# Attention, routed experts and a gated MLP on one core: where a cast load and five gathers stand on GpSimd's queue, the order of row numbers and tables, and the first slot's rows by blocks of 128

## The chip, the cores and the metric

The kernel runs on one core of one Trainium2 chip. The metric is the device time of one execution in microseconds (us); less is better. Engines are called as in the profile: PE is TensorE (its weight loads are PEld), DVE is VectorE, ACT is ScalarE, POOL is GpSimd, SP is SyncE. A q behind a name (POOLq, SPq) is the queue in which that engine issues DMAs.

## The reference

Three layers, all in float32, with 4 batches of 576 tokens:

```python
# 1. attention with a threshold, 8 heads of 64
scores = scale * q @ k.T
scores = where(scores >= max(scores) - tau, scores, -1e9)
x = softmax(scores) @ v                       # reshaped to [2304, 512]
# 2. each token goes to one of 8 experts (512 -> 1024 -> 512)
logits = norm(x) @ norm(expert_emb).T / moe_tau
e = argmax(logits);  gate = softmax(logits)[e]
y = gate * (relu(x @ w1[e]) @ w2[e])
# 3. a dense layer with a mish gate (512 -> 2048 -> 512)
h = y @ w_in;  out = (h * tanh(softplus(h))) @ w_out
```

## The kernel before, in words

**Stages.** By the trace, attention runs to about 294 us, routing to about 323 us, the experts to about 660 us, and the dense layer to the end.

**Slots.** Routing sorts the 2304 tokens by expert into slots of 128 rows. There are SLOTS = 25 of them; with these inputs the experts 0 to 7 begin at slots 0, 2, 5, 7, 9, 12, 15 and 19. The number of each row is worked out on DVE and PE (`sel`, `tid`, a matmul over 18 tiles into the bank at INV0) and becomes `inv_i` (L1437 and L1438). POOL then fetches the rows of each slot from `x_tok` in DRAM by an indirect DMA, `gather(s)` (L629).

**One slot on PE** (`slot(i)`): `m1(i)`, 24 blocks of matmuls of 512 columns in all (2 halves, 4 blocks of k, 3 passes: high x high, high x low, low x high; L1111 to L1113), then `t_x(i + 1)`, four transposes of the next slot's rows (L1107), then `m2(i - 1)` (24 matmuls), then `t_h(i)` (8 transposes). The three passes are how float32 products are formed from float32r operands: each operand is a high part (a copy into float32r) and a low part (the difference). For the rows, ACT makes `xth` (`high_x`, L840) and DVE makes `xtl` (`low_x`, L1484).

**The weights.** Each expert's weights have 16 chunks of 128x512 in 4 quarters; quarters 0 and 1 are w1, 2 and 3 are w2. The high part comes by a casting DMA of 1 MB, `load_quarter(e, par, i)` (L603), issued by POOL. The low part needs the raw chunk too: SP loads it into one of 4 `stage` buffers (L475), each once POOL has used that buffer's chunk before (`w_split`), and POOL subtracts (`low_quarter`, `low_parts`, L592). There are two sets of buffers for the high parts, so expert e's quarters 0 and 1 may load once all m1 of expert e - 2 are done, and its quarters 2 and 3 once all m2 of it are.

**The order on POOL** behind attention is written out by hand: the cast loads of expert 1's quarters 1 to 3, low parts of its quarters 1 and 2, the 15 gathers of slots 0 to 14 (they wait for `placed`), 3 gathers that wait for `gates_kept` (the slots' gates, written by DVE at L1477 when PE has done the matmuls of `gsel`, L1163), and then for each expert e from 2 on `next_expert(e)`:

```python
wait m1_done (all slots before expert e - 1)
load_quarter(e, 0);  load_quarter(e, 1)
if e == 2: gather(18), gather(19)
low_quarter(e - 1, 3);  low_quarter(e, 0)
wait m2_done (all slots before expert e - 1)
load_quarter(e, 2);  load_quarter(e, 3)
low_quarter(e, 1);  low_quarter(e, 2)
```

Between `next_expert(2)` and `next_expert(3)` stand the 5 gathers of slots 20 to 24. PE's `m1` of an expert's slots waits for `w_split` of its first 8 chunks, the last of which is the end of `low_quarter(e, 1)`.

**ps** is PSUM: 8 banks of 512 columns. The transposed rows of a slot go to columns 0 to 511, `m1` writes 512 to 1535, `t_h` 1536 to 2559, `m2` 2560 to 3071.

Of the kernel before, what the change touches and what calls it, by code (L numbers as in the profile page):

```python
# [16 lines left out]
ALU = mybir.AluOpType  # L17
ACT = mybir.ActivationFunctionType
# [57 lines left out]
HEAD = 4  # L76
YW = D + 1
# [5 lines left out]
def build(nc, qT, kT, v, tau, embT, moe_tau, w1, w2, w_in, w_out, out):  # L83
# [335 lines left out]

    LG0 = 2048  # L420
# [107 lines left out]
    def _(g):  # L528
# [93 lines left out]
        for i in range(1, QUARTERS):  # L622
            load_quarter(1, 1, i)
        for i in range(1, 3):
            low_quarter(1, 1, 1, i)

# [15 lines left out]
        def next_expert(e, par, n):  # L642

            first = g.value_load(start_i[0:1, bass.ds(e - 1, 1)], min_val=1, max_val=SLOTS)
            g.wait_ge(m1_done, g.snap(first * 2))
            g.sem_inc(pool_passed, 1)
            load_quarter(e, par, 0)
            load_quarter(e, par, 1)
            if isinstance(e, int) and e == 2:
                for s in range(FAR, AHEAD):  # L650
                    gather(s)
            low_quarter(e - 1, 1 - par, n - 1 + par, 3)
            low_quarter(e, par, n, 0)
            g.wait_ge(m2_done, first)
            g.sem_inc(pool_passed, 1)
            load_quarter(e, par, 2)
            load_quarter(e, par, 3)
            low_quarter(e, par, n, 1)
            low_quarter(e, par, n, 2)

        next_expert(2, 0, 2)
        for s in range(AHEAD, SLOTS):
            gather(s)
# [90 lines left out]
    def _(act):  # L754
# [82 lines left out]
        def high_x(i):  # L837
            act.wait_ge(tx_done, i + 1)
# [33 lines left out]
        high_x(0)  # L872
# [58 lines left out]
    def _(pe):  # L931
# [160 lines left out]
        def t_x(i):  # L1092
# [11 lines left out]
            wait(pe, xth_ready, i)  # L1104
            wait(pe, xtl_ready, i)
# [12 lines left out]
        def m1(i, e):  # L1118
            pe.wait_ge(w_split, e * CH_E + CH_E // 2)
            pe.wait_ge(xtl_ready, i + 1)  # L1120
            par = pe.snap(e % 2)
            for h in range(2):
                wait(pe, relu_done, 2 * i - 1 + h)
                for k in range(KD):
                    o = k * F + h * 512
# [133 lines left out]
    def _(dve):  # L1259
# [169 lines left out]
        for t in range(NT):  # L1429
            dve.tensor_scalar(sel[:, t, :], lane_b[:, :], prow[:, t:t + 1], None, ALU.is_equal).then_inc(sel_ready, 1)  # L1430
        dve.tensor_copy(start_i[:, :], start[:, :])
# [4 lines left out]
        dve.wait_ge(inv_mm, 1)  # L1436
        link(dve.tensor_copy(idp[:, :], ps[:, INV0:INV0 + SLOTS]))  # L1437
        dve.scalar_tensor_tensor(inv_i[:, :], ps[:, INV0 + SLOTS:INV0 + 2 * SLOTS], float(P), idp[:, :], ALU.mult,  # L1438
                                 ALU.add).then_inc(placed, 1)
# [41 lines left out]
        def low_x(i):  # L1481

            dve.wait_ge(xth_ready, i + 1)
# [26 lines left out]
        low_x(0)  # L1510
# [110 lines left out]
```

## Time and profile before

| | |
|---|---|
| time of 3 runs | 1074.81, 1074.88, 1077.37 us; median 1074.88 us |
| profiled execution | 1076.51 us, of which the span of instructions is 1074.9 us |
| PE busy | 1026.1 us, 95% of the span |
| DVE, ACT, POOL busy | 627.3, 505.8, 587.3 us |
| mean granted PE clock | 0.982 of 2.4 GHz |

The time of the profiled execution is 1.6 us longer than its span, and 1.6 us longer than the median of the three runs. Busy shares say where an engine works, not where it holds up the end; a row that ends in [t <-X] says that the engine sat idle for t before it and that X ended this.

### The profile page before, as it was taken

To read this page: it belongs to the slowest core of one execution; us is meant where nothing else is said; L and a number is where in the kernel's file an instruction comes from. 1 tells how busy PE (TensorE), PEld (TensorE's weight loads), DVE (VectorE), ACT (ScalarE), POOL (GpSimd) and SP (SyncE) were. 2 spreads that over 40 slices of the span, in tenths; PEclk is the share of its full clock that TensorE was granted. 3 is DMA by queue.
4 is the path that set the end of the run, shared out by engine and by line. 5 is a ranking of instruction groups with operands and counts; after the bars stand their busy time and mean duration, and the time that the engine had idled before them with its cause. 6 is when DMAs were issued, how large, how long until landed. Compare 5 with 4: busy or idle time off the path is not lost.

```text
span 1074.9 us, 20987 instructions
## 1 busy us (share of the span) xinstructions
PE 1026.1 (95%) x6712; PEld 852.0 (79%) x6712; DVE 627.3 (58%) x1484; ACT 505.8 (47%) x1020; POOL 587.3 (55%) x672
## 2 busy tenths in 40 slices
PE   7999999999956999899999998999999999999996
PEld 5777777777735888688888887999999999999995
DVE  6998989888763222122222226766676676666663
ACT  5777777777652222122222223454545545555542
POOL 3345445444346768767750717766556565565564
PEclk9999999999988999999999998999999999999998
DMA  8155424441065899889872746200000000000000
GB/s 200 39 165 160 129 83 138 130 120 44 12 218 157 273 286 290 260 292 283 264 226 99 227 141 188 73 30 21 13 28 30 30 10 20 29 29 0 11 20 30
DMA packets 97526, 128.87 MB, mean 120 GB/s; under 512 B 34400, under 2 KB 51808, under 8 KB 96928
## 3 DMA queue, kind: packets, MB, share of 16 engines
q1 hardware_dynamic: 72544, 66.54, 21.6%
q0 software_dynamic: 18880, 53.22, 15.6%
q10 hardware_dynamic: 6016, 7.96, 2.1%
q8 instruction: 53, 0.87, 0.4%
q14 instruction: 33, 0.27, 0.1%
HBM read 111.70 MB, written 16.00 MB: 119 GB/s over the span
## 4 chain that ended last, share of the span: by engine, by line
PE 59%; POOL 4%; DMA 4%; issue 2%; DVE 2%; ACT 1%; another core or an unknown queue 1%; POOLq 0%; SPq 0%; DVEq 0%; ACTq 0%
PE ps L1111 18%; PE ps L1113 18%; PE ps L1112 18%; DMA stage<-w 4%; POOL wl L592 3%; PE ps L1137 1%; PE ps L1049 1%; PE ps L1186 1%; POOL wh L603 1%; PE ps L1107 1%; POOL xs_far L629 1%; PE ps L1059 1%; ACT junk L825 1%; POOL out L686 0%
## 5 line engine op out<-in xcount | busy, mean ns | idle before, releaser
L592 POOL TENSOR_TENSOR wl<-stage,wh 128x512 fp32r<-128x512 f32 x128 | 163.0, 1295 | 58.0 <-DMA stage<-w 51.8
L711 POOL TENSOR_TENSOR mg<-mw,mr 128x384 f32<-128x384 f32 x96 | 116.8, 1217 | 76.0 <-DVE mr L1546 75.7
L767 ACT ACTIVATE ex<-sc,rmin 128x576 f32<-128x576 f32 x144 | 111.6, 776 | 78.4 <-DVE sc L1317 78.4
L717 POOL TENSOR_TENSOR gl<-mg,gh 128x384 fp32r<-128x384 f32 x96 | 98.6, 1027 | 78.9 <-ACT gh L903 78.9
L1111 PE MATMUL ps<-yth,winh 128*128 128x384 f32 x384 | 131.0, 341 | 0.0
L1113 PE MATMUL ps<-yth,winl 128*128 128x384 f32 x384 | 129.5, 337 | 0.0
L1112 PE MATMUL ps<-ytl,winh 128*128 128x384 f32 x384 | 128.8, 335 | 0.0
L1327 DVE SCALAR_TENSOR_TENSOR pm<-sc,thr,ex 128x576 f32<-128x576 f32 x144 | 116.7, 812 | 19.2 <-POOL thr L556 15.3
L1317 DVE TENSOR_SCALAR_CACHE_REDUCE sc<-ps,nscale 128x576 f32<-128x576 f32 x144 | 116.9, 814 | 10.1 <-PE ps L958 9.3
L1111 PE MATMUL ps<-wouth,gh 128*128 128x512 f32 x288 | 113.8, 395 | 4.8 <-DVE yo L1491 4.8
L556 POOL TENSOR_SCALAR thr<-rmin,taup 128x1 f32<-128x1 f32 x144 | 75.4, 524 | 76.6 <-DVE sc L1317 74.6
L1112 PE MATMUL ps<-woutl,gh 128*128 128x512 f32 x288 | 114.2, 396 | 0.0
L1113 PE MATMUL ps<-wouth,gl 128*128 128x512 f32 x288 | 112.6, 391 | 0.0
L1523 DVE TENSOR_SCALAR mm<-ps 128x384 f32<-128x384 f32 x96 | 53.3, 555 | 90.9 <-PE ps L1113 90.8
L895 ACT ACTIVATE ml<-mn,two 128x384 f32<-128x384 f32 x96 | 59.3, 617 | 99.0 <-DVE mn L1527 99.0
L1484 DVE TENSOR_TENSOR xtl<-ps,xth 128x512 fp32r<-128x512 f32 x25 | 17.3, 691 | 130.7 <-ACT xth L840 125.2
L1006 PE MATMUL ps<-pt,vb 128*64 128x128 f32 (+1 forms) x1280 | 93.4, 282 | 0.0
L891 ACT ACTIVATE mm<-mm 128x384 f32<-128x384 f32 x96 | 50.3, 524 | 91.5 <-DVE mm L1523 90.8
L1111 PE MATMUL ps<-wh,xth 128*128 x200 | 82.2, 411 | 7.0 <-POOL wl L592 5.1
L958 PE MATMUL ps<-k_t,q_t 64*128 64x288 f32 x512 | 82.1, 440 | 6.0 <-DMA k_t<-kT 6.0
L855 ACT ACTIVATE hth<-ps 128x512 fp32r<-128x512 f32 x50 | 27.2, 596 | 127.8 <-PE ps L1137 121.1
L1006 PEld LDWEIGHTS ps<-pt,vb 128*64 128x64 f32 (+1 forms) x1280 | 67.0, 135 | 21.6 <-issue 21.6
(193 smaller groups left out, 2256.6 us busy)
## 6 DMA issues: line engine op xcount, KB each, us to landing
stage<-w SPq DMA_DIRECT2D x128, 256.0 KB, 4.6
wh<-w POOLq DMA_DIRECT2D x32, 1024.0 KB, 8.6
y_dense<-yo ACTq DMA_DIRECT2D x25, 256.5 KB
q_t<-qT SPq DMA_DIRECT2D x16, 288.0 KB, 3.7
k_t<-kT SPq DMA_DIRECT2D x16, 288.0 KB, 4.0
vb<-v SPq DMA_DIRECT2D x16, 288.0 KB, 4.6
stage<-w_in SPq DMA_DIRECT2D x16, 256.0 KB, 3.4
winh<-w_in POOLq DMA_DIRECT2D x1, 4096.0 KB, 14.0
```

What stands on the lines that cost most here:

```text
L556: g.tensor_scalar(thr[:, i % 2, t:t + 1], rmin[:, i % 2, t:t + 1], taup[:, :], None, ALU.add).then_inc(thr_ready, 1)
L592: g.tensor_tensor(dst, raw, src.bitcast(F32), ALU.subtract).then_inc(w_split, 1)
L711: g.tensor_tensor(mg[:, f % 2, :], mw[:, f % 2, :], mr[:, f % 2, :], ALU.mult).then_inc(g_done, 1)
L717: g.tensor_tensor(gl[:, f % 4, :], mg[:, f % 2, :], gh[:, f % 4, :].bitcast(F32), ALU.subtract).then_inc(gl_ready, 1)
L767: act.activation(ex[:, i % 2, t * S:(t + 1) * S], sc[:, i % 2, t * S:(t + 1) * S], ACT.Exp, bias=rmin[:, i % 2, t:t + 1], scale=-1.0).then ...
L958: m = pe.matmul(s_psum(lane)[:, h, :], q_t[st // HEADS][rows, st % HEADS, q0:q0 + P], k_t[rows, st, h * S // 2:(h + 1) * S // 2], start=Tr ...
L1006: m = pe.matmul(ps[to, OT0:OT0 + P], vb[rows, st, k, :], pt[rows, i % 2, k * P:(k + 1) * P], start=c == 0, stop=c == PAIRS)
L1111: pe.matmul(out_, lhs_h, rhs_h, start=start, stop=False)
L1112: pe.matmul(out_, lhs_h, rhs_l, start=False, stop=False)
L1113: return pe.matmul(out_, lhs_l, rhs_h, start=False, stop=stop)
L1317: dve.tensor_scalar(sc[:, i % 2, t * S:(t + 1) * S].rearrange("p (h n) -> p h n", h=2), s_psum(t), nscale[:, :], BIG, ALU.mult, ALU.min, a ...
L1327: dve.scalar_tensor_tensor(pm[:, i % 2, t * S:(t + 1) * S], sc[:, i % 2, t * S:(t + 1) * S], thr[:, i % 2, t:t + 1], ex[:, i % 2, t * S:(t ...
```

## The change

Four edits, and nothing else of the work changes.

1. On POOL, the cast load of expert 1's quarter 3 (1 MB) moves from ahead of the low parts of its quarters 1 and 2 to behind them.
2. On DVE, the two instructions that make `inv_i` (the row numbers) move ahead of the four that make the tables `start_i` and `sexp_i`.
3. Slot 0's four transposes go into four different banks and signal one by one; ACT and DVE make `xth` and `xtl` of each block of 128 as it comes, and PE's first `m1` waits block by block. The semaphores count 3 more from then on (`MORE`).
4. On POOL, the 5 gathers of slots 20 to 24 move from ahead of `next_expert(3)` to behind its first two cast loads, so also behind its wait for `m1_done` and ahead of its low parts.

```diff
@@ -74,6 +74,7 @@
 NG = NT // GT_
 LAG = 4
 HEAD = 4
+MORE = KD - 1
 YW = D + 1
 TY = 7
 
@@ -417,6 +418,10 @@
         a = 3072 + 512 * (k % 2) if isinstance(gi, int) and gi == 0 else 3584
         return ps[:, a:a + GW]
 
+    def x0_psum(k):
+        a = (0, 1536, 2048, 2560)[k]
+        return ps[:, a:a + P]
+
     LG0 = 2048
     Z0 = 3072
     INV0 = 3584
@@ -619,10 +624,11 @@
         for b in range(NITER):
             attention(b)
         g.wait_ge(normed, NUNIT)
-        for i in range(1, QUARTERS):
+        for i in range(1, 3):
             load_quarter(1, 1, i)
         for i in range(1, 3):
             low_quarter(1, 1, 1, i)
+        load_quarter(1, 1, 3)
 
         def gather(s):
             got = x_first[s] if s < FIRST else x_near if s < NEAR else x_far if s < FAR else x_next if s < AHEAD else x_last
@@ -646,8 +652,8 @@
             g.sem_inc(pool_passed, 1)
             load_quarter(e, par, 0)
             load_quarter(e, par, 1)
-            if isinstance(e, int) and e == 2:
-                for s in range(FAR, AHEAD):
+            if isinstance(e, int) and e in (2, 3):
+                for s in range(FAR, AHEAD) if e == 2 else range(AHEAD, SLOTS):
                     gather(s)
             low_quarter(e - 1, 1 - par, n - 1 + par, 3)
             low_quarter(e, par, n, 0)
@@ -659,8 +665,6 @@
             low_quarter(e, par, n, 2)
 
         next_expert(2, 0, 2)
-        for s in range(AHEAD, SLOTS):
-            gather(s)
         next_expert(3, 1, 2)
         with g.Fori(2, E // 2) as b:
             for par in range(2):
@@ -835,7 +839,7 @@
         act.wait_ge(gate_ln, 1)
         act.activation(nr1[:, :], nr0[:, :], ACT.Exp, scale=0.5).then_inc(gate_ln, 1)
         def high_x(i):
-            act.wait_ge(tx_done, i + 1)
+            act.wait_ge(tx_done, i + 1 + MORE)
             wait(act, m1_done, 2 * i)
             act.activation(xth[:, :, :], ps[:, 0:512], ACT.Copy).then_inc(xth_ready, 1)
 
@@ -869,7 +873,9 @@
 
         act.wait_ge(gate_in, 1)
         act.activation(lg3[:, :, :], lg2[:, :, :], ACT.Exp).then_inc(gate_exp, 1)
-        high_x(0)
+        for k in range(KD):
+            act.wait_ge(tx_done, k + 1)
+            act.activation(xth[:, k, :], x0_psum(k), ACT.Copy).then_inc(xth_ready, 1)
         slot(0, True)
         act.wait_ge(dst_set, 1)
         with act.Fori(1, SLOTS - 2) as i:
@@ -1101,8 +1107,12 @@
             elif i == AHEAD:
                 pe.wait_ge(x_last, 16 * (SLOTS - AHEAD))
             rows = x_slot(i)
-            wait(pe, xth_ready, i)
-            wait(pe, xtl_ready, i)
+            if i == 0:
+                for k in range(KD):
+                    pe.transpose(x0_psum(k), rows[:, k * P:(k + 1) * P], ident[:, :]).then_inc(tx_done, 1)
+                return
+            pe.wait_ge(xth_ready, i + MORE)
+            pe.wait_ge(xtl_ready, i + MORE)
             for k in range(KD):
                 t = pe.transpose(hx[:, k * P:(k + 1) * P], rows[:, k * P:(k + 1) * P], ident[:, :])
             t.then_inc(tx_done, 1)
@@ -1117,11 +1127,14 @@
 
         def m1(i, e):
             pe.wait_ge(w_split, e * CH_E + CH_E // 2)
-            pe.wait_ge(xtl_ready, i + 1)
+            if i > 0:
+                pe.wait_ge(xtl_ready, i + 1 + MORE)
             par = pe.snap(e % 2)
             for h in range(2):
                 wait(pe, relu_done, 2 * i - 1 + h)
                 for k in range(KD):
+                    if i == 0 and h == 0:
+                        pe.wait_ge(xtl_ready, k + 1)
                     o = k * F + h * 512
                     m = passes(ps[:, 512 * (1 + h):512 * (2 + h)], xth[:, k, :], xtl[:, k, :],
                                wh_f[:, bass.ds(par * (CH_E * CHUNK) + o, 512)],
@@ -1428,15 +1441,15 @@
                           ALU.mult).then_inc(id_t, 1)
         for t in range(NT):
             dve.tensor_scalar(sel[:, t, :], lane_b[:, :], prow[:, t:t + 1], None, ALU.is_equal).then_inc(sel_ready, 1)
+        dve.wait_ge(inv_mm, 1)
+        link(dve.tensor_copy(idp[:, :], ps[:, INV0:INV0 + SLOTS]))
+        dve.scalar_tensor_tensor(inv_i[:, :], ps[:, INV0 + SLOTS:INV0 + 2 * SLOTS], float(P), idp[:, :], ALU.mult,
+                                 ALU.add).then_inc(placed, 1)
         dve.tensor_copy(start_i[:, :], start[:, :])
         link(dve.tensor_tensor(scmp[:, :, :], sidx[:, :, :],
                                start[:, 1:E].unsqueeze(1).to_broadcast([P, SLOTS, E - 1]), ALU.is_ge))
         link(dve.tensor_reduce(sexp[:, :], scmp[:, :, :], AX.X, ALU.add))
         dve.tensor_copy(sexp_i[:, :], sexp[:, :]).then_inc(routed, 1)
-        dve.wait_ge(inv_mm, 1)
-        link(dve.tensor_copy(idp[:, :], ps[:, INV0:INV0 + SLOTS]))
-        dve.scalar_tensor_tensor(inv_i[:, :], ps[:, INV0 + SLOTS:INV0 + 2 * SLOTS], float(P), idp[:, :], ALU.mult,
-                                 ALU.add).then_inc(placed, 1)
         link(dve.scalar_tensor_tensor(waste[:, :], nslot[:, 1:E + 1], float(P),
                                       incl[:, :, NT - 1], ALU.mult, ALU.subtract))
         link(dve.tensor_tensor(scmp[:, :, :], scmp[:, :, :],
@@ -1480,7 +1493,7 @@
 
         def low_x(i):
 
-            dve.wait_ge(xth_ready, i + 1)
+            dve.wait_ge(xth_ready, i + 1 + MORE)
             dve.tensor_tensor(xtl[:, :, :], ps[:, 0:512].rearrange("p (k t) -> p k t", k=KD),
                               xth[:, :, :].bitcast(F32), ALU.subtract).then_inc(xtl_ready, 1)
 
@@ -1507,7 +1520,10 @@
                                   hth[:, 4 * h:4 * h + 4, :].bitcast(F32), ALU.subtract).then_inc(htl_ready, 1)
 
         gate_logits()
-        low_x(0)
+        for k in range(KD):
+            dve.wait_ge(xth_ready, k + 1)
+            dve.tensor_tensor(xtl[:, k, :], x0_psum(k), xth[:, k, :].bitcast(F32),
+                              ALU.subtract).then_inc(xtl_ready, 1)
         gates()
         slot(0, True)
         with dve.Fori(1, SLOTS - 1) as i:
```

## Rows read from the trace of the kernel before

**Rows 1.** The page: busy time of PE, its share of the span, instructions.

```profile
PE 1026.1 (95%) x6712; PEld 852.0 (79%) x6712; DVE 627.3 (58%) x1484; ACT 505.8 (47%) x1020; POOL 587.3 (55%) x672
```

**Rows 2.** PE's waits over the span: who for whom, us, times, longest.

```profile
PE ps L1111 <- POOL wl L592: 5.1, 1, 5.1
PE ps L1111 <- DVE yo L1491: 4.8, 1, 4.8
```

**Rows 3.** Timeline where expert 4 begins: start, us, engine, line, instruction.

```profile
445.79 0.79 PE L1111 MATMUL ps<-wh,xth 128*128 x1 [5.10 <-POOL wl L592]
...
449.48 0.39 PE L1111 MATMUL ps<-wh,xth 128*128 x1
```

**Rows 4.** Timeline of POOL from the last gathers through expert 3's loads.

```profile
383.39 1.09 POOL L629 DMA_INDIRECT xs_far<-x_tok,inv_i  x1 [0.16 <-issue]
...
389.73 1.55 POOL L603 DMA_DIRECT2D wh<-w  x2
391.23 5.14 POOL L592 TENSOR_TENSOR wl<-stage,wh 128x512 fp32r<-128x512 f32 x4
400.04 1.30 POOL L592 TENSOR_TENSOR wl<-stage,wh 128x512 fp32r<-128x512 f32 x1 [3.68 <-DMA stage<-w]
...
407.11 1.52 POOL L603 DMA_DIRECT2D wh<-w  x2
```

**Rows 5.** Timeline of ACT and DVE: what follows slot 4's m1 and m2.

```profile
384.57 0.60 ACT L847 ACTIVATE hs<-ps 128x512 f32<-128x512 f32 x1 [2.07 <-issue]
...
403.05 0.15 DVE L1490 COPY yo<-inv_i 128x1 int32 x1 [4.30 <-PE ps L1113]
```

**Rows 6.** Stages: length, busy us (count) by engine, PEclk, DMA share, GB/s.

```profile
389.00:396.00 7.00, 7.00 (x36) 5.85 (x35) 2.06 (x4) 1.69 (x3) 7.00 (x7) 1.00 0.90 212
396.00:404.00 8.00, 8.00 (x43) 6.68 (x42) 1.64 (x4) 1.83 (x4) 2.29 (x3) 1.00 1.00 357
```

**Rows 7.** Timeline of POOL and DVE during routing.

```profile
308.83 2.50 POOL L592 TENSOR_TENSOR wl<-stage,wh 128x512 fp32r<-128x512 f32 x2 [0.20 <-DMA stage<-w]
...
310.09 1.41 DVE L1401 TENSOR_TENSOR lg<-z,lmax 128x144 f32<-128x144 f32 x1
```

**Rows 8.** Timeline of POOL and DVE in the dense layer.

```profile
668.89 0.79 POOL L693 DMA_DIRECT2D wouth<-w_out  x1
...
670.93 1.03 POOL L711 TENSOR_TENSOR mg<-mw,mr 128x384 f32<-128x384 f32 x1
```

**Rows 9.** Timeline of DVE at the same place.

```profile
668.99 3.40 DVE L1527 SCALAR_TENSOR_TENSOR mn<-mm 128x384 f32<-128x384 f32 x1 [0.95 <-ACT mm L891]
```

**Rows 10.** Timeline: row numbers, and the first gather.

```profile
318.38 2.90 PE L1084 MATMUL ps<-tid,sel 128*128 128x50 bf16 x18 [4.93 <-DVE sel L1430]
...
321.81 0.18 DVE L1437 COPY idp<-ps 128x25 f32<-128x25 f32 x1
...
323.17 1.14 POOL L629 DMA_INDIRECT xs_near<-x_tok,inv_i  x1 [11.84 <-ACT junk L825]
```

**Rows 11.** Timeline: slot 0's rows, and a DVE operation ahead of them.

```profile
325.58 0.31 DVE L1452 TENSOR_TENSOR lg<-lg,rn 128x144 f32<-128x144 f32 x1
...
326.77 1.08 PE L1107 MATMUL ps<-ident,xs_near 128*128 128x128 f32 x4 [5.49 <-DMA xs_near<-x_tok,inv_i]
...
329.53 0.79 PE L1111 MATMUL ps<-wh,xth 128*128 x1 [1.68 <-DVE xtl L1484]
```

**Rows 12.** ACT's copy of 128 columns in attention: duration min/median/max.

```profile
L784 ACT ACTIVATE ot<-ps x70: 267/268/278, 22.9 to 289.4; 128x128 f32<-128x128 f32 x70
```

**Rows 13.** Timeline behind slot 0's m1.

```profile
337.20 0.82 PE L1163 MATMUL ps<-gsel,sel 128*128 128x75 bf16 x18
...
344.01 0.39 PE L1113 MATMUL ps<-wh,xtl 128*128 x1 [1.62 <-issue]
...
344.91 1.09 ACT L855 ACTIVATE hth<-ps 128x512 fp32r<-128x512 f32 x2 [6.72 <-remote]
...
346.25 1.00 POOL L629 DMA_INDIRECT xs_far<-x_tok,inv_i  x1 [3.27 <-DVE gslot L1477]
```

## The prediction

> **What bounds the kernel.** Read the page first: PE is busy for 95% of the span [rows 1]. So a change can only win where PE still waits, or where its clock is low. PE's waits come next. Two of them matter here: 5.1 us for POOL's low parts of weights and 4.8 us for `yo` near the end [rows 2]. The first stands at 445.79 us, at the first slot of expert 4 (slot 9), and PE has no wait for POOL behind it [rows 2, 3]. So this is the gate of the whole expert stage: what PE gains ahead of it is lost in the wait, and what POOL's chain gains up to it moves all that follows, until PE itself is the bound there. It holds 5.1 us. Behind the wait the first matmul stands with 0.79 us and 3.7 us later one stands with 0.39 [rows 3]: half clock, then full clock.
>
> Then follow POOL back from the gate. At 383.39 it starts five gathers, at 389.73 it issues expert 3's first two cast loads, and at 391.23 it makes four low parts. It then waits 3.68 us for a stage load, starts the next four at 400.04 and gets to expert 3's other loads at 407.11 [rows 4]. While the gathers are issued the loads could already run; instead they begin 6.34 us late and then compete with the stage loads.
>
> **Edit 4, the gathers behind the loads.** The loads now wait for the last m1 ahead of expert 2's end, slot 4. ACT starts on its result at 384.57 [rows 5], so this is when the wait ends; before, the gathers hid it. The five gathers cost POOL the 6.34 us they cost now (389.73 - 383.39), the loads 1.50 (391.23 - 389.73), four low parts 5.14 [rows 4]. With nothing else moved: 384.6 + 1.5 + 6.3 + 5.1 = 397.5 for the end of the first four low parts, and 402.7 for the next four if their chunks are there. What is queued behind the new wait are the gathers (slot 20 is far away) and expert 2's last low parts, 1.2 us later than before (397.5 against 396.4), which slot 5's m2 needs; it can't start before slot 4's has ended, at 403.05 [rows 5]: covered.
>
> Are the chunks there? SP reloads a buffer when POOL has used it, from about 393.7 on. By then 2 MB of loads and 1.3 MB of gathers, started at 384.6, are under way. The rate of DMA was 212 GB/s where gathers and loads met and 357 where loads and stage chunks ran [rows 6]. At 212 some 1.4 MB are still queued at 393.7, at 357 almost none. So the residual wait is between 0 and about 3 us; I take 0.8, as the low rate also holds the issue time of the gathers. That makes the end 403.5 and the gain at 407.11 3.6 us. The following wait, for slot 4's m2, ends at 403.05 [rows 5]: just covered. If both edges were bad (3 us more), the gain is 0.6.
>
> **Edit 1, the cast load behind the low parts.** It saves no work. It takes 1 MB out of the way of the stage chunks that POOL waits for, so that POOL's last two low parts of that stretch, now 308.83 to 311.33 [rows 7], end about 1.6 us earlier (1 MB at the 357 GB/s is 2.9 us, of which half is in front of them). This matters through DVE: its subtraction with two SBUF inputs at 310.09 took 1.41 us, until 311.50 [rows 7], while one of the same size took 0.31 with no subtraction on POOL [rows 11]. It ends when POOL's work does. Another such case is worse: a DVE operation begun at 668.99 took 3.40 us, from POOL's issue of a cast load until the end of POOL's subtraction at 671.96 [rows 8, 9]. So POOL's moved issue, 0.75 us, can hold DVE too. Bounds of the edit: 1.1 us of routing (1.41 - 0.31) if the issue falls clear, 0.3 if it falls on the operation. I take 0.7. The load itself lands long before the gathers; its user is at 354.
>
> The Trainium skill, "SBUF — State Buffer", section "SBUF: two separate sides", says that DVE and GpSimd share a port pair as an exclusive lock held for a whole instruction, by a DVE operation with two SBUF inputs too. The two rows agree; by that rule the gain would be the same 0.7.
>
> **Edit 2, row numbers first.** PE's matmuls end at 321.28 and the copy starts only at 321.81 [rows 10], as the tables are made in between. Now it can follow at once: 0.5 us, less 0.05 for the semaphore; I take 0.45, bounds 0.3 and 0.5. The tables come 0.4 us later, and their first reader waits for rows from DRAM until 326.77 [rows 11]. Edits 1 and 2 together move the first gather from 323.17 to 322.0, by 1.15.
>
> **Edit 3, blocks.** From the first transpose to the first matmul it takes 2.76 us now (326.77 to 329.53) [rows 11]. By blocks: a quarter of the transposes (0.3), ACT's copy of 128 columns (0.27) [rows 12], DVE's subtraction of about that size (0.31) [rows 11], three hand-overs as now (0.4 to 0.5): 1.35, so 1.4 us saved; nothing if only the last block counted. It costs ACT and DVE three more instructions each, about 0.6 us, beside PE's slow matmuls. But all of this is PE time ahead of the gate: it helps only if POOL is no longer late there.
>
> **The start of POOL's chain.** Behind slot 0, ACT sits idle for 6.72 us and starts at 344.91, though the matmuls of the gates, just ahead of the transposes it waits for, are recorded by 338.0; PE pauses 1.62 us itself, and POOL's next gather waits 3.27 us until 346.25 [rows 13]. I don't know what holds this; it ends soon after the last of the 15 gathers, issued by 342.98 (346.25 - 3.27). If it goes with the gathers, everything moves by their 1.15 us. Bounds: 0 if it stays put, about 4.4 if it vanishes (3.27 + 1.15). I take 1.15.
>
> **The sum.** POOL reaches expert 3's gate 1.15 earlier, and so does PE's slot 4. 3.6 + 1.15 = 4.75 us at the gate of expert 4; PE, 1.15 earlier, is there at 439.5, POOL at 441.0. PE's wait is then about 1.5 us. The clock: behind a pause of 1.62 us the matmul took 0.39, full clock [rows 13], but behind 5.10 it was half [rows 3]. With 1.5 us I expect no fall, which gives back 7.5 matmuls x (0.43 - 0.23) = 1.5 us. Total 6.25: the profiled execution, 1076.5, would be at 1070.3. The median of the runs is 1.6 us below that execution, and it may be that they had less of the low clock to lose; against 1074.9 the sum is 4.75 to 6.25. I predict 1069.5 us (5.4 less). The late wait of 4.8 us for `yo` is bound to PE's own work and moves with it [rows 2]; its clock can fall otherwise than now, 1 to 3 us either way.
>
> The Trainium skill, "TensorE: Matmul & The Clock Gate", section "What's actually happening", has the clock follow recent activity; here 1.62 us idle did not lower it and 5.10 did, and no row lies between. By that rule alone the 1.5 us would be likely but not sure, and the sum 4.75 without it.
>
> **Rivals.** (a) The gathers' rate decides: expert 3's first chunks wait behind 3.3 MB at 212 GB/s or less, edit 4 gives only 0.6, and the whole gain is 1.15 + 0.6 = 1.75 to 3: 1072 to 1073. For it: the 212. Against: the gathers are issued over 6.3 us, so 212 may be the rate of their issue and no limit of the engines. Chance 0.2. (b) The hold behind slot 0 vanishes, as the work around it is moved: POOL then starts 4.4 earlier, and the gate's wait is gone altogether, the rest being PE's: 7.5 to 10 us, 1065 to 1067.4. For it: nobody visible holds it. Chance 0.12. (c) No change: POOL's wait for slot 4's m1 and the later low parts eat what the loads win, and the 0.75 us issue lands on DVE: within 1 us of before. Chance 0.1. (d) Slower, by one mechanism: stage chunks starve at 393 to 410. 3.3 MB and then 1 MB must be through, from 383.5 on, before POOL makes the last low part (1.3 us) of those that now end at 407.1. That leaves 22.3 us: it is slower below 193 GB/s. At 160 it would take 26.9 us and end at 411.7, 4.6 late: 1079. Against: 357 GB/s at 396 to 404 [rows 6]. Chance 0.06. The forecast keeps 0.52, with a range of its own of 1067.5 to 1071.5.
>
> **Numbers.** 0.3% is 3.2 us, about what a measurement tells from none. Faster than 1071.7: nearly all of the forecast, (b), and a third of (a): 0.7. Slower than 1078.1: 0.06. Range over (a) to (b): 1066 to 1073.3.
>
> **What would show it.** After: the cast loads at L603 of expert 3 stand ahead of the gathers, near 383.5, and the low parts' wait for `stage` near 400 is under 1.5 us; PE's wait at slot 9 is 0 to 2 us, and the matmuls behind it take 0.39; DVE's L1401 analogue takes 0.3 to 1.0; the first gather starts near 322.0; the first m1 starts 1.35 behind the first transpose. I am wrong if a stall of POOL on `stage` grows by over 3 us, if POOL's wait for m1 grows, or if a wait of PE comes up at slots 5 to 8.

## The result: slower by 0.37%

The changed kernel takes 1079.2 us (median of 21 executions) where the kernel before takes 1074.9 (21): ratio 1.0037, 95% interval 1.0024 to 1.0051. The forecast was 1069.5. The profiled execution of the changed kernel took 1079.7 us, with a span of 1078.1, 3.2 us longer than the span of before.

Read the same views in the same order. The page's busy times and PE's waits (who for whom, us, times, longest):

```profile
PE 1028.9 (95%) x6712; PEld 854.4 (79%) x6712; DVE 626.2 (58%) x1487; ACT 506.1 (47%) x1023; POOL 586.0 (54%) x672
```

```profile
PE ps L1121 <- POOL wl L597: 5.8, 1, 5.8
...
PE ps L1121 <- DVE yo L1504: 4.8, 1, 4.8
```

The gate did not open. PE's wait for POOL has grown from 5.1 us [rows 2] to 5.8; the forecast had it at 1.5. The timeline of PE at that place:

```profile
448.76 0.79 PE L1121 MATMUL ps<-wh,xth 128*128 x1 [5.82 <-POOL wl L597]
...
452.33 0.40 PE L1123 MATMUL ps<-wh,xtl 128*128 x1
```

It stands 2.97 us later than in [rows 3], which is the whole loss in span (3.2) but for 0.2. Half clock lasts 3.6 us behind it and lasted about as long before (3.5 us, 445.79 to 449.25), so the clock gave nothing back either. Now POOL's chain to the gate, the stretch of [rows 4]:

```profile
378.43 5.16 POOL L597 TENSOR_TENSOR wl<-stage,wh 128x512 fp32r<-128x512 f32 x4 [3.12 <-DMA stage<-w]
387.39 1.49 POOL L608 DMA_DIRECT2D wh<-w  x2 [3.80 <-PE ps L1123]
389.18 1.07 POOL L635 DMA_INDIRECT xs_far<-x_tok,inv_i  x1 [0.30 <-issue]
...
395.53 5.05 POOL L597 TENSOR_TENSOR wl<-stage,wh 128x512 fp32r<-128x512 f32 x4
406.13 5.07 POOL L597 TENSOR_TENSOR wl<-stage,wh 128x512 fp32r<-128x512 f32 x4 [5.56 <-DMA stage<-w]
411.13 1.59 POOL L608 DMA_DIRECT2D wh<-w  x2
```

Take as a yardstick the stretch from POOL's last low part of expert 2's quarter 2 (here 378.43 + 5.16 = 383.59) to the issue of expert 3's later loads: 27.54 us. Before it was 407.11 - 383.23 = 23.88 (the gathers began 0.16 after that end). The forecast's value is 23.9 - 3.6 = 20.3. Two rows hold the 7.2 us between: the wait for slot 4's m1 is 3.80 where 1.4 was taken (384.6 - 383.2), and the wait for `stage` is 5.56 where 0.8 was. The rest of the stretch is as costed.

Against the kernel before the comparison comes out otherwise. There POOL waited for `stage` twice in this stretch, 3.68 us at 400.04 [rows 4] and then once more:

```profile
403.37 3.81 POOL L592 TENSOR_TENSOR wl<-stage,wh 128x512 fp32r<-128x512 f32 x3 [2.03 <-DMA stage<-w]
```

Together these are 5.71 us, and the change has 5.56. So the wait for `stage` has not grown; it has not shrunk either, which the forecast counted on. What makes the stretch 3.66 us longer than before is the wait for slot 4's m1, 3.80 us where there was none.

What was the DMA doing? Windows (length, busy us by engine, granted clock, DMA share, GB/s), and under them the view of DMA for the second one:

```profile
389.00:396.00 7.00, 7.00 (x37) 5.83 (x36) 2.16 (x4) 1.09 (x2) 5.58 (x6) 1.00 1.01 355
396.00:404.00 8.00, 8.00 (x39) 6.58 (x38) 0.69 (x1) 1.72 (x3) 4.57 (x4) 1.00 0.75 186
```

```profile
q0 software_dynamic: 280, 0.89, 54.3%
q1 hardware_dynamic: 176, 0.34, 12.5%
...
stage<-w SPq DMA_DIRECT2D x4, 256.0 KB, 8.1
```

Compare [rows 6]. The order is reversed: first 355 GB/s, while the 2 MB of cast loads and 0.4 MB of the gathers run (2.49 MB in all); then 186, when the last gather has been issued (394.51 to 395.51) and POOL's queue has only packets of gathers left. So 186 is not the rate of the issue. The queue of POOL moved 0.89 MB in 54.3% of the 8 us, 205 GB/s of its own time, and SP's queue 0.34 MB in 12.5%, 340 GB/s. And the last column: the stage chunks that POOL waits for land 8.1 us after their issue. Those of the kernel before, issued at 389 to 396, did little better:

```profile
stage<-w SPq DMA_DIRECT2D x3, 256.0 KB, 7.1
```

### The profile page after: what moved, and what is told of

Same layout as the page of the kernel before. It is cut to its first block, busy times and chain, and to the rows that moved or that the text cites. A ratio compares the mean times of both kernels' runs of the same rounds, so it can differ in the third digit from the quotient of the medians.

```text
span 1078.1 us, 20993 instructions
## 1 busy us (share of the span) xinstructions
PE 1028.9 (95%) x6712; PEld 854.4 (79%) x6712; DVE 626.2 (58%) x1487; ACT 506.1 (47%) x1023; POOL 586.0 (54%) x672
## 4 chain that ended last, share of the span: by engine, by line
PE 63%; DMA 3%; POOL 3%; issue 2%; DVE 1%; ACT 1%; another core or an unknown queue 0%; POOLq 0%; SPq 0%; DVEq 0%; ACTq 0%
PE ps L1121 19%; PE ps L1122 19%; PE ps L1123 19%; DMA stage<-w 3%; PE ps L1150 2%; POOL wl L597 2%; PE ps L1055 1%; PE ps L1117 1%; PE ps L1199 1%; PE ps L1065 1%; ACT junk L829 0%; DMA xs_near<-x_tok,inv_i 0%; POOL xs_far L635 0%; POOL wh L608 0%
## 5 line engine op out<-in xcount | busy, mean ns | idle before, releaser
L721 POOL TENSOR_TENSOR gl<-mg,gh 128x384 fp32r<-128x384 f32 x96 | 98.2, 1023 | 78.4 <-ACT gh L909 78.4
L851 ACT ACTIVATE hs<-ps 128x512 f32<-128x512 f32 x50 | 29.9, 598 | 119.4 <-PE ps L1123 109.3
```

Of the source, the lines that this page charges most:

```text
L721: g.tensor_tensor(gl[:, f % 4, :], mg[:, f % 2, :], gh[:, f % 4, :].bitcast(F32), ALU.subtract).then_inc(gl_ready, 1)
```

## The experiments

All ratios are against the kernel before on the same chip, with 95% intervals. "Stretch" is the yardstick above, and the three columns behind it are what POOL waits in it: for slot 4's m1, for `stage`, and for slot 4's m2. "Gate" is the end of the low parts for which PE waits at slot 9. All of these are read from the timeline of one execution, while the ratios are of 6 to 21 executions. The chips are numbered as on record; that of the first two rows is not on record.

| kernel | chip | ratio | stretch | m1 | stage | m2 | gate | PE's wait there |
|---|---|---|---|---|---|---|---|---|
| before | | | 23.9 | 0 | 5.7 | 0 | 445.6 | 5.1 |
| the change | | 1.0037 (1.0024 to 1.0051) | 27.5 | 3.8 | 5.6 | 0 | 448.6 | 5.8 |
| only4 | 5 | 1.0029 (1.0008 to 1.0051) | 25.6 | 3.2 | 4.2 | 0 | 443.2 | 4.9 |
| only3 | 5 | 1.0025 (1.0003 to 1.0048) | 23.0 | 0 | 4.8 | 0 | 440.1 | 4.0 |
| only3_b | 1 | 1.0023 (1.0006 to 1.0041) | 24.0 | 0 | 5.8 | 0 | 442.7 | 6.9 |
| no4 | 5 | 0.9998 (0.9978 to 1.0019) | 23.8 | 0 | 5.7 | 0 | 439.0 | 4.0 |
| no3 | 5 | 1.0015 (0.9994 to 1.0037) | 25.5 | 3.0 | 4.3 | 0 | 440.6 | 5.0 |
| edits12 | 12 | 0.9992 (0.9973 to 1.0011) | 23.6 | 0 | 5.5 | 0 | 444.0 | 5.4 |
| burst10 | 12 | 1.0022 (1.0005 to 1.0038) | 23.7 | 0 | 5.6 | 0 | 447.7 | 6.1 |
| late | 12 | 0.9941 (0.9920 to 0.9962) | 20.1 | 1.8 | 2.5 | 4.2 | 439.6 | 0.3 |
| late12 | 12 | 0.9931 (0.9906 to 0.9955) | 20.3 | 2.0 | 2.4 | 4.3 | 437.1 | none |
| late12_b | 1 | 0.9967 (0.9952 to 0.9982) | 22.0 | 3.7 | 2.2 | 4.5 | 437.7 | 0.2 |
| mid4 | 13 | 0.9977 (0.9961 to 0.9993) | 21.7 | 3.5 | 0 | 0 | 438.7 | 0.9 |
| plain4 | 13 | 0.9963 (0.9946 to 0.9981) | 21.8 | 3.6 | 3.1 | 0.8 | 438.4 | 0.9 |
| late123 | 13 | 0.9929 (0.9906 to 0.9952) | 19.6 | 1.3 | 3.7 | 3.0 | 434.6 | none |
| late123_b | 1 | 0.9942 (0.9922 to 0.9962) | 18.3 | 0 | 3.1 | 3.5 | 435.1 | none |
| before_look | 13 | (one execution) | 22.7 | 0 | 4.5 | 0 | 440.3 | 2.1 |
| change_look | 1 | (one execution) | 24.4 | 1.5 | 4.7 | 0 | 441.0 | 5.0 |

**Which edit does it?** Each edit by itself, or left out, by the hunks of the diff above. `only4` is edit 4 alone:

> Edit 4 alone on the kernel before: the five last gathers behind expert 3's first two cast loads. Theory G (gathers): while the gathers' packets run, the stage chunks of expert 3 do not land, so POOL's wait for stage near 400 us is 5 us or more against 3.7, POOL reaches expert 3's later loads at or behind 407, the wait of PE at slot 9 stays at 5 us or more, and the time is 1 to 4 us above before. Theory B (blocks): the loss of the whole change comes from edit 3, through slot 4's m1 being 2.2 us late; with edit 4 alone the cast loads start at 385 and the time is 2 to 5 us below before.

1.0029: edit 4 alone makes the kernel slower. Its POOL:

```profile
382.50 1.50 POOL L603 DMA_DIRECT2D wh<-w  x2 [3.19 <-PE ps L1111]
...
399.69 2.54 POOL L592 TENSOR_TENSOR wl<-stage,wh 128x512 fp32r<-128x512 f32 x2 [4.00 <-DMA stage<-w]
...
404.92 1.59 POOL L603 DMA_DIRECT2D wh<-w  x2
```

The same two waits, 3.19 and 4.00, with none of the other edits in the kernel. Theory G had expected 5 us or more for `stage`, against 3.7; it was 4.20 in all, against 5.71, so what is added is again the wait for m1. `only3` is edit 3 alone, and `no4` edits 1 to 3:

> Edit 3 alone: the first slot by blocks of 128. Theory B: slot 1's m1 ends at 349 to 350 instead of 347.5, the clock falls to half at about 340, and the lateness gets through to the gate at slot 9: 1 to 4 us above before. Theory G: slot 1's m1 ends late as well, but POOL's loads of expert 3 do not wait for it (the gathers hide that wait), the gate stays at 445.8 within 1 us, and the time is that of before within 1.5 us.

> The changed kernel without edit 4 (edits 1, 2 and 3). Theory G: the loss is gone, within 1.5 us of before. Theory B: 2 to 5 us above before, as the whole change.

`only3` is slower too, 1.0025. Theory B had forecast that, but through a late m1 of slot 1 and a later gate; the gate stood at 440.1, and `no4`, which B had at 2 to 5 us above before, is as before. So B's way is not what makes it slower. `no3` is edits 1, 2 and 4:

> The changed kernel without edit 3 (edits 1, 2 and 4). Theory G: as edit 4 alone, 1 to 4 us above before, with POOL's wait for stage at 5 us or more. Theory B: 2 to 5 us below before. If both edits are needed for the loss (the late m1 of slot 4 makes the loads late, and only then do the gathers meet the stage chunks), both this and edit 3 alone are within 1.5 us of before.

1.0015, not told apart from no change; it has edit 4's stretch (25.5) with its wait for m1 (2.98), and PE's wait at the gate is 5.0.

**Is it the gathers' place?** `late` takes edit 4's purpose further: the five gathers go behind expert 7's last low parts, where slot 20 is still ahead.

```diff
         next_expert(2, 0, 2)
-        for s in range(AHEAD, SLOTS):
-            gather(s)
         next_expert(3, 1, 2)
...
         low_quarter(E - 1, 1, E // 2, 3)
+        for s in range(AHEAD, SLOTS):
+            gather(s)
```

> The kernel before, but the five last gathers stand behind all low parts of expert 7, where POOL waits 27 us for PE anyway; no other edit. Theory G (while gathers' packets run, stage chunks and all other transfers are late, and the wait for slot 4's m1 is no longer hidden): with no gathers there, POOL waits about 3 us for slot 4's m1, then under 2 us for stage, reaches expert 3's later loads 3 us or more earlier than before, and is then held by slot 4's m2. PE's wait at slot 9 is 1 to 3 us. Time 2 to 5 us below before. Rival (rate): the DMA engines are the limit over the whole chain, so the gathers' 1.3 MB gone gives 1.3 MB at 357 GB/s, 3.6 us at most at the gate, and not all of it. Rival (nothing): the chain is bound by PE's m1 and m2 of slot 4 and the time is that of before within 1 us.

0.9941: 0.59% is 6.3 us, and the medians lie 7.1 us apart (1069.14 against 1076.22), more than the 2 to 5 us expected. POOL, and the view of DMA over 386 to 396:

```profile
383.97 1.48 POOL L603 DMA_DIRECT2D wh<-w  x2 [1.84 <-PE ps L1113]
385.47 5.04 POOL L592 TENSOR_TENSOR wl<-stage,wh 128x512 fp32r<-128x512 f32 x4
392.99 5.07 POOL L592 TENSOR_TENSOR wl<-stage,wh 128x512 fp32r<-128x512 f32 x4 [2.48 <-DMA stage<-w]
402.21 1.51 POOL L603 DMA_DIRECT2D wh<-w  x2 [4.16 <-PE ps L1113]
```

```profile
stage<-w SPq DMA_DIRECT2D x6, 256.0 KB, 4.6
```

Without gathers the chunks land in 4.6 us, not 8.1, POOL's wait for `stage` is 2.48 us, the stretch is 20.1 us, and 4.16 of it is now a wait for PE: POOL is ahead of PE. PE no longer stops at the gate:

```profile
439.79 0.49 PE L1111 MATMUL ps<-wh,xth 128*128 x1 [0.30 <-POOL wl L592]
```

**Is it the bytes or the kind of transfer?** `mid4` puts the gathers one step later than edit 4, behind the low parts of expert 2's quarter 3. So SP can issue the next stage chunks before the gathers.

```diff
             load_quarter(e, par, 1)
...
             low_quarter(e - 1, 1 - par, n - 1 + par, 3)
+            if isinstance(e, int) and e == 3:
+                for s in range(AHEAD, SLOTS):
+                    gather(s)
             low_quarter(e, par, n, 0)
```

> Edit 4 with another place: the five gathers behind expert 3's first cast loads and behind expert 2's last low parts, ahead of expert 3's first. The stage chunks are then asked for ahead of the gathers. Theory G (gather packets in the queues keep the stage chunks from landing): the wait for stage ahead of expert 3's first low parts all but goes (under 1.5 us), as the gathers cover it; from the end of expert 2's quarter 2 to the issue of expert 3's later loads it takes about 3 + 1.5 + 5.1 + 6.3 + 5.1 = 21 to 23 us, against 23.6 in kernels without edit 4 and 25.5 to 27.5 with it; time 1 to 3 us below before. Rival (total traffic): the chunks land when all of the traffic has gone through, wherever the gathers stand: 25 us or more, and the time of edit 4 alone, 1.003 of before.

0.9977. The gathers are the same, only four low parts later:

```profile
382.51 1.50 POOL L603 DMA_DIRECT2D wh<-w  x2 [3.46 <-PE ps L1114]
384.03 5.03 POOL L592 TENSOR_TENSOR wl<-stage,wh 128x512 fp32r<-128x512 f32 x4
389.23 1.08 POOL L629 DMA_INDIRECT xs_far<-x_tok,inv_i  x1 [0.17 <-issue]
...
395.60 5.04 POOL L592 TENSOR_TENSOR wl<-stage,wh 128x512 fp32r<-128x512 f32 x4
400.76 1.59 POOL L603 DMA_DIRECT2D wh<-w  x2
```

There is no wait for `stage` at all: the chunks come in while the gathers are being issued. Both signs of theory G came (under 1.5 us of that wait, a stretch of 21 to 23). `plain4` keeps edit 4's place and its bytes and changes the kind (its output is not the reference's):

```diff
         def gather(s):
+            if s >= AHEAD:
+                g.dma_start(x_slot(s), x_tok[(s - AHEAD) * P:(s - AHEAD + 1) * P, :]).then_inc(got, 16)
+                return
```

> Edit 4, with the gathers of slots 20 to 24 replaced by plain loads of the same size from consecutive rows of x_tok, issued at the same place on the same queue; slot 20 then works on other tokens' rows, so the output is not the reference's. Theory G (what is special is the gathers: their packets run at 190 to 210 GB/s and the rest waits): with plain loads the bytes pass at 350 GB/s or more, the chunks land 3 us sooner after their issue, the span from expert 2's quarter 2 to expert 3's later loads falls below 22 us and the time is 2 us or more below before. Rival (bytes): the same bytes stand in front of the chunks, the wait for stage stays at 3 us or more, and only the cheaper issue on POOL (5 x 0.5 us) is won.

0.9963, and this is edit 4's order. POOL, and DMA over 386 to 396:

```profile
383.57 2.72 POOL L630 DMA_DIRECT2D xs_far<-x_tok  x5
386.30 5.06 POOL L592 TENSOR_TENSOR wl<-stage,wh 128x512 fp32r<-128x512 f32 x4
394.46 5.07 POOL L592 TENSOR_TENSOR wl<-stage,wh 128x512 fp32r<-128x512 f32 x4 [3.10 <-DMA stage<-w]
400.35 1.53 POOL L603 DMA_DIRECT2D wh<-w  x2 [0.82 <-PE ps L1114]
```

```profile
DMA packets 1466, 3.97 MB, mean 397 GB/s; under 512 B 183, under 2 KB 183, under 8 KB 1465
...
q0 software_dynamic: 762, 2.66, 71.1%
...
stage<-w SPq DMA_DIRECT2D x5, 256.0 KB, 5.7
```

The DMA engines move 397 GB/s here, all queues together. In the second part of that window, 390 to 394, the 2 MB of cast loads are through, and POOL's queue moves 1.01 MB of the plain loads in 67.0% of 4 us, 377 GB/s of its own time. The chunks land after 5.7 us. What this is worth to POOL is less clear. Against `only4`, the same kernel but for the kind of transfer, the stretch is 3.8 us shorter, and 3.6 of that is issue time (2.72 us where the gathers took 6.35); the wait for `stage` is 3.10 against 4.20, and 0.82 us of waiting for PE came in its place. The rival (bytes) had named a wait of 3 us or more as its sign. So the rates are told apart, while what `plain4` gains in the stretch is mostly its cheaper issue.

**The first two edits, and a shorter burst.** `edits12` is edits 1 and 2. `burst10` issues 10 gathers ahead of the wait for `gates_kept` in place of 15, and the other 8 behind it.

> Edits 1 and 2 alone. First gather 0.3 to 1.2 us earlier than in the kernel before, as is the gate at slot 9; time 0.3 to 1.5 us below before. If DVE's blocked operations are only exchanged (the low parts still end near 311), it is edit 2's 0.4 us alone.

0.9992, no difference, where 0.3 to 1.5 us had been expected.

```diff
+BURST = 10
...
-        for s in range(NEAR):
+        for s in range(BURST):
             gather(s)
         g.wait_ge(gates_kept, 1)
-        for s in range(NEAR, FAR):
+        for s in range(BURST, FAR):
             gather(s)
```

> The kernel before, but only slots 0 to 9 are gathered ahead of gates_kept, and slots 10 to 17 behind it. Theory H (the late signals of PE behind slot 0 last while the row of gathers runs): the hold ends by about 339 in place of 344.8, or does not appear. Then POOL's chain behind the gates starts no earlier, as five gathers more (6.5 us) stand in it: the gate at slot 9 within 2 us of before, or up to 4 us later if the gathers in front of expert 2's loads push the stage chunks. If the hold has nothing to do with the gathers, it stays at 337 to 345.

1.0022: slower. The hold behind slot 0 (ACT and DVE idle for up to 6.7 us on results that PE has by the records finished [rows 13]) is absent from its trace, and yet the gate is at 447.7: with eight gathers behind the gates, POOL's waits for `stage` at expert 2 are 4.15 and 3.59 us (before: 3.52, then 1.28 and 2.00), and it begins the stretch 1.9 us later. One execution without the hold fits theory H, but does not show it.

**Without the gate.** `late12` adds edits 1 and 2 to `late`, and `late123` edits 1 to 3.

> As the kernel with the late gathers, with edits 1 and 2 as well. Edits 1 and 2 move the first gather by 0.4 to 1.2 us earlier and so POOL's chain; with the late gathers the gate is no longer POOL's alone, so 0 to 1 us below the late gathers alone.

> Edits 1, 2 and 3 with the late gathers, so all of the change but with the gathers in POOL's idle time instead of behind expert 3's loads. With POOL no longer late at the gate, PE's own time counts: the blocks' 1.4 us should show, at the gate of slot 4 and to the end, as 0.5 to 1.5 us below edits 1 and 2 with late gathers (0.9931 of before). If the late signals of PE behind slot 0 end when the gathers end, whatever PE did before, the blocks bring nothing: within 0.5 us of that kernel.

0.9931 and 0.9929; `late12` is 1.4 us below `late` by the medians, on the same chip, where 0 to 1 had been expected. `late12` and `late123` were measured on different chips; on one chip:

> Edits 1 and 2 with late gathers, now on the same chip as the next kernel, which has edit 3 as well. Reference for it; 0.992 to 0.995 of before.

> Edits 1, 2 and 3 with late gathers. Without a wait for POOL at slot 9, what the blocks win in front should reach the end: 1 to 2 us below the kernel with edits 1 and 2 and late gathers. If the blocks bring nothing even without the gate, both agree within 0.5 us.

1066.95 and 1065.49 us, the kernel before being at 1070.55. Between their medians lie 1.46 us, and edit 3 was costed at 1.4. The intervals of the two ratios overlap, but both kernels ran on one chip, and seven of the eleven executions of `late123_b` are below the lowest of the twelve of `late12_b` (1065.93). So edit 3 is worth something there, and its size agrees. `late123` is the fastest kernel of all: 0.9929 and 0.9942.

**Why is edit 3 alone slower?** `before_look` is one execution of the kernel before, `only3_b` repeats `only3`, and `change_look` is one more execution of the whole change.

> The kernel before once more, with a profile: whether the late signals of PE behind slot 0 (ACT idle for 6.7 us at 338 to 345) are there in each execution. If they belong to the kernel, they are there again; if they come and go by execution or chip, they may be missing, POOL then starts its chain at 343 and not at 346, and this is part of the spread of the times.

> Edit 3 alone once more. Theory C (clock): the blocks bring PE to slot 9 earlier by 1 to 2 us, POOL's chain stays, so PE's wait there grows to 3.5 us or more and the clock falls behind it, where the kernel before often waits only 2 us with no fall: 0 to 3 us above before, with few or no runs in the kernel before's fast group (the 1068 to 1070 us of the earlier chip). Rival: the loss measured first was chance, and the ratio is 0.998 to 1.000.

> The whole change once more, with a profile, on a chip where PE's late signals behind slot 0 may be missing. Theory G: also without them it takes 25 us or more from the end of expert 2's quarter 2 to the issue of expert 3's later loads, with a wait for m1 near 3 us and a wait for stage of 4 us or more, and PE waits 5 us or more at slot 9 with the clock at half behind it. If the loss of the whole change hangs on the late signals, the wait at slot 9 is under 3 us.

`only3_b` is slower again (1.0023). PE at the gate, first in `before_look`, then in `only3_b`:

```profile
440.45 0.50 PE L1111 MATMUL ps<-wh,xth 128*128 x1 [2.14 <-POOL wl L592]
...
441.33 0.39 PE L1111 MATMUL ps<-wh,xth 128*128 x1
```

```profile
442.86 0.79 PE L1122 MATMUL ps<-wh,xth 128*128 x1 [6.94 <-POOL wl L597]
...
446.75 0.39 PE L1122 MATMUL ps<-wh,xth 128*128 x1
```

In `before_look` PE idles for 2.14 us and its clock stays up; in `only3_b` it idles for 6.94 and the next 3.9 us are at half clock. PE is ready 2.4 us earlier (435.92 against 438.31) and the gate stands 2.4 us later. Edit 3 brings PE to a gate that POOL does not open earlier, so it lengthens the pause. Then the clock falls more often, which costs 1.4 us each time: the first half of slot 9's m1 ends 4.7 us behind the gate with the fall and 3.3 without. The executions of the kernel before form two groups on the chip of `only3`, 15 of them at 1067.6 to 1070.1 us and 20 at 1071.7 to 1076.3, while the lowest of `only3`'s twelve is 1071.2. The granted clock on record fits that: 0.983 or more in 12 of the 15, and in none of the 20, of the 12 of `only3` or of the 12 of `only3_b`. That the groups are those without and with the fall at slot 9 stays an argument, as only few executions have a timeline. 1.4 us is less than the distance of the groups, so something else must go with it.

`change_look`, at 1071.89 us, has edit 4's waits once more, 1.50 for m1 and 4.66 for `stage`, its gate at 441.0, and a wait of PE of 5.02 us with half clock behind it. Its stretch is 24.4, not 25 or more, and its wait for m1 is half of what was expected. But PE's wait is not under 3 us, so it does not hang on the hold.

## Why the prediction was wrong

**The bound was right.** The gate at slot 9 sets the time: of the 3.2 us lost in span it carries 2.97, and `late`, which opens it, is 6.3 us faster.

**Edit 4, the step that failed**: "The residual wait is between 0 and about 3 us; I take 0.8, as the low rate also holds the issue time of the gathers." It was 5.56, and 4.20, 4.30 and 4.66 in `only4`, `no3` and `change_look`, above even my upper bound. The step took for granted that cast loads issued ahead of the gathers would shorten POOL's waits for `stage`. They were 5.71 before and 4.5 to 5.8 in the six other traces with the gathers at the old place, so edit 4 left them about as they were.

I took 212 GB/s of [rows 6] for the rate of the issue. But in the change 186 GB/s stands where no gather is issued any more. And the 212 was itself a mean of two things: the last gather was issued by 389.74, but POOL's queue moved only 0.25 MB from 391 to 393, in 98.2% of the time, and the GB/s rose to 421 only behind 394, when the 1.3 MB of gathers were through. So in both orders packets of gathers were still running while SP's chunks for POOL's next low parts were wanted: before until 394, in the change until 404. The change has only turned round which of the two, gathers or cast loads, goes first. Per byte the gathers' packets took 1.8 times as long as those of plain loads (205 GB/s of the queue's own time in the change against 377 in `plain4`), and in other windows with only gathers in POOL's queue more than twice as long (127 in the kernel before, 131 in `mid4`).

**Slot 4's m1.** "ACT starts on its result at 384.57" was taken as fixed, a wait of 1.4 us. It was 3.80, and 3.2 to 3.6 in `only4`, `mid4` and `plain4`. In the last three POOL is 4 to 5 us earlier there (its stretch starts at 378.5 to 379.3) and m1 only 2, so POOL meets it sooner; in the change m1 itself is 2.8 us later, most of it (2.2) lost behind slot 0. The five gathers, ahead of this wait, filled it: their 6.34 us of issue covered a wait that edit 4 lays bare. The gain counted them as pure delay but for 1.4 us. These two terms, 2.4 + 4.8, are the 7.2 us between forecast and measured stretch; against the kernel before this wait alone makes the loss. The four traces of the old order without the hold (`before_look`, `only3`, `only3_b`, `no4`) have stretches of 22.7 to 24.0, the three of edit 4 without it 24.4 to 25.6.

**The rivals.** Rival (d) forecast 1079 and 1079.2 came, by luck: its mean rate from 383.5 to 405.8 was 241 GB/s in the change, above its limit of 193 (the 186 is of 8 us of that), and the chunks starved no more than before. Its counter-evidence was none either: in the 357 GB/s of [rows 6] no gather ran. The wait that decided, for slot 4's m1, is named in rival (c), with 0.1, and it ate more than (c) gave it.

**The clock** was to give back 1.5 us at a pause of 1.5. That pause was mis-added: PE's arrival at 439.5 holds edits 1 and 2 but not the 1.4 us of edit 3, with which it would be 438.1, and the pause 2.9. Single pauses of 1.62, 2.14 and 3.10 us (the last in `burst10`, at slot 7) left the clock up, and behind 4.01, 5.1, 5.8 and 6.9 it stood at half; so it did behind two of 1.79 and 1.55 with 0.8 us of transposes between them (the change, 341.71, shown below). Its price was right in size (1.4), but with the gathers at the old place or at edit 4's the pause at slot 9 never came under 2.14. The Trainium skill, "TensorE: Matmul & The Clock Gate", section "What's actually happening", has the clock follow recent activity; the rows agree.

**Edits 1 and 2.** From the copy of `lgt_l` to the first gather it took 15.38 us before and 15.24 in the change, a gain of 0.14 where 1.15 was taken. Edit 2 gave its 0.5: the copy follows the end of PE by 0.04 us (321.47 to 321.51) and not by 0.53. Edit 1 lost 0.34. DVE and POOL in routing:

```profile
309.93 0.80 DVE L1414 TENSOR_TENSOR lg<-z,lmax 128x144 f32<-128x144 f32 x1
310.76 1.26 DVE L1415 SCALAR_TENSOR_TENSOR lg<-lg,desc 128x144 f32<-128x144 f32 x1
```

```profile
306.92 1.26 POOL L597 TENSOR_TENSOR wl<-stage,wh 128x512 fp32r<-128x512 f32 x1 [0.97 <-DMA stage<-w]
309.30 2.56 POOL L597 TENSOR_TENSOR wl<-stage,wh 128x512 fp32r<-128x512 f32 x2 [1.11 <-DMA stage<-w]
```

POOL's low parts ended at 311.86, no earlier than before (311.33), as the chunks were late, and they held two DVE operations in place of one. In `no4` the same edit does as forecast, with POOL's issue of the load right beside DVE:

```profile
309.33 0.31 DVE L1416 TENSOR_TENSOR lg<-z,lmax 128x144 f32<-128x144 f32 x1
309.68 0.31 DVE L1417 SCALAR_TENSOR_TENSOR lg<-lg,desc 128x144 f32<-128x144 f32 x1
```

```profile
306.99 2.49 POOL L597 TENSOR_TENSOR wl<-stage,wh 128x512 fp32r<-128x512 f32 x2 [0.59 <-DMA stage<-w]
309.43 0.77 POOL L608 DMA_DIRECT2D wh<-w  x1
```

There the gain is 1.6 us (13.80 against 15.38). What decides is whether the chunks come in time, and that differs between executions; in `edits12` they did too (13.67). But nothing of it reaches the end while POOL is bound later (0.9992).

**Edit 3** was costed well. From the first transpose to the first matmul it takes 1.41 us, forecast 1.35:

```profile
326.55 1.09 PE L1112 MATMUL ps<-ident,xs_near 128*128 128x128 f32 x4 [5.08 <-DMA xs_near<-x_tok,inv_i]
327.96 0.79 PE L1121 MATMUL ps<-wh,xth 128*128 x1 [0.32 <-DVE xtl L1525]
```

"It helps only if POOL is no longer late there" was right as well. That it would hurt if POOL is late, through a longer pause and the clock, I did not see.

**The start of POOL's chain.** The hold behind slot 0 came back larger in the change; ACT and PE there:

```profile
338.69 0.60 ACT L851 ACTIVATE hs<-ps 128x512 f32<-128x512 f32 x1 [4.82 <-remote]
...
344.60 1.08 ACT L859 ACTIVATE hth<-ps 128x512 fp32r<-128x512 f32 x2 [3.87 <-remote]
```

```profile
339.34 0.82 PE L1150 MATMUL ps<-ident,hs 128*128 128x128 f32 x4 [1.79 <-ACT hs L851]
...
341.71 0.79 PE L1121 MATMUL ps<-wh,xth 128*128 x1 [1.55 <-issue]
```

Slot 1's m1 ended at 349.75 (before: 347.53), 2.2 us later, though its chain began 1.6 earlier. POOL's chain did not start 1.15 earlier: its next gather stands at 345.93 [rows 13: 346.25], and the load behind it then waits 0.84 for PE. What the hold is stays open. It is there in `before`, the change, `late`, `late12` and `edits12`, and absent from the thirteen other traces, among them `before_look`, the same kernel as before, and `change_look`, the same as the change. So it does not go with an edit. It may go with the chip: three of the four traces of chip 12 have it (`burst10`, with its shorter burst, has not), and none of the twelve of chips 5, 13 and 1. The kernel before had its highest median on chip 12 (1076.2, against 1072.6, 1071.7 and 1070.6), which fits a loss of some us there but is no proof. It also bears on the gain of the late gathers: edits 1 and 2 with them won 8.5 us by the medians on chip 12 and 3.6 on chip 1, so the 6.3 us of `late` are of a chip with the hold. The forecast used the hold as if it belonged to the kernel.

**What was shown and what not.** Shown: that edit 4 alone makes the kernel slower, and that POOL then waits for slot 4's m1 (four traces of three kernels, and no trace of the old order) while its wait for `stage` stays; that gathers run slower than plain loads of the same bytes; that gathers behind the experts' loads open the gate. Argued only: how much of the time comes from that wait, as each stretch is of one execution; the share of the hold and of the clock in each execution, and so why the whole change (1.0037) lies above `only4` (1.0029) and `no3` (1.0015), whose intervals overlap.

## What to carry to other kernels

Before issue time is moved, write down which wait it covers at its old place and which at its new one. Here 6.3 us of issue ahead of POOL's wait for m1 hid that wait; behind it, and ahead of low parts that had their chunks, the issue hid nothing (POOL's waits in the stretch: 5.7 us before, 9.4 in the change); one step later it hid the wait for `stage` (3.5 in `mid4`). A transfer that nobody needs for over 150 us paid best behind the last wait of the bound chain (`late`). Write down as well what still runs in the DMA engines when the slow engine needs its next chunk: the end of the issue is not the end of the packets. And while one gate is closed, shortening the work ahead of it can cost: it lengthens a pause, and here the clock fell for it; open the gate first, and the same edit pays (1.5 us between the medians of `late12_b` and `late123_b`).

## What was new of the hardware

- Gathers of 128 rows of 2 KB took the DMA queue at 205 GB/s of its own time in the change, 127 in a window of the kernel before and 131 in one of `mid4`; plain loads of the same bytes at 377. Chunks of 256 KB in SP's queue landed 8.1 (the change), 7.3 (`only4`) and 7.1 us (before) behind their issue beside gathers, 5.7 beside plain loads and 4.6 in `late`. The Trainium skill, "DMA: Bandwidth & Descriptors", section "Queues, rings and completion order", has an engine take its queues in turn by packets. That fits with chunks that get on, if slowly; how the turn is shared is not shown by these runs.
- While the first gathers ran, ACT sat idle for up to 6.7 us on results of PE that the records have as done, in one execution of the kernel before and of the change and not in another of the same kernel.
- POOL's issue of a cast load beside DVE operations with two SBUF inputs did not hold them (0.31 us each), while POOL's subtractions did (0.80 and 1.26). In the dense layer of the kernel before, a DVE operation begun during such an issue ended only behind the two POOL operations that followed it (3.40 us) [rows 8, 9], so the issue alone is not cleared by these rows, and the prediction's "the two rows agree" is safe for [rows 7] only.
